# Two-scale attention and two feed-forward layers: first layer in tiles of 288 and 432 tokens, attention pairs in five or six chunks

## The reference

```python
# attention, batch 4, heads 8, seq 576, head_dim 64, all float32
out_d = softmax_attention(mean of 4 tokens of q, k, v)         # 144 x 144 scores per head
out_local = softmax_attention(q, k, v, masked to |i - j| < 4)  # a band around the diagonal
x = repeat(out_d, 4) + out_local                               # -> 2304 tokens x 512
# layer 1: w_in 512 x 2048, w_out 2048 x 512
h = x @ w_in;  x = maximum(0.01 * h, h) @ w_out
# layer 2, weights of the same shapes
h = x @ w_in2; out = (h - tanh(h)) @ w_out2
```

## Time and profile before

| what | us |
|---|---|
| three runs | 952.02, 952.35, 954.28 |
| the profiled execution's own time | 951.99 |
| its span, first to last instruction | 950.2 |
| around the span | 1.8 |
| PE matmul busy | 939.5 |
| layer 1, first to last | 42.98 to 541.24 |

### The profile page before, as it was taken

How to read it: one execution, slowest core, us unless ns; L and a number is a source line. 1 busy time by engine, 2 the same in 40 slices (tenths; PEclk the granted TensorE clock), 3 DMA queues, 4 the chain that set the end, 5 groups by cost and what they waited for, 6 DMA issues and landing times.

```text
span 950.2 us, 19922 instructions
## 1 busy us (share of the span) xinstructions
PE 939.5 (99%) x7026; PEld 883.6 (93%) x7026; DVE 529.2 (56%) x1070; ACT 557.0 (59%) x1351; POOL 403.5 (42%) x343
## 2 busy tenths in 40 slices
PE   8999999999999999999999999999999999999998
PEld 8799999999999999999999989889899898898997
DVE  6744434534543554344236576776666766766764
ACT  5756446445445455463446677665765755755754
POOL 4776428236246164171534567333233233233232
PEclk9999999999999999999999999999999999999999
DMA  7875211210121121102004022000000000000000
GB/s 159 190 200 141 53 27 27 51 44 26 31 51 26 25 51 45 34 1 68 1 2 143 3 67 78 34 1 1 34 0 0 33 0 0 33 0 0 34 1 33
DMA packets 87797, 41.48 MB, mean 44 GB/s; under 512 B 60352, under 2 KB 81344, under 8 KB 87744
## 3 DMA queue, kind: packets, MB, share of 16 engines
q1 hardware_dynamic: 87744, 40.78, 16.3%
HBM read 36.04 MB, written 4.72 MB: 43 GB/s over the span
## 4 chain that ended last, share of the span: by engine, by line
PE 88%; ACT 4%; POOL 3%; DVE 2%; DMA 1%; issue 1%; SPq 0%; ACTq 0%; DVEq 0%; POOLq 0%
PE ph L540 13%; PE ph L542 13%; PE ph L541 13%; PE acc L569 7%; PE acc L571 7%; PE acc L570 7%; PE acc L616 6%; PE acc L617 6%; PE acc L618 6%; PE banks L429 2%; PE banks L466 2%; PE banks L453 1%; PE banks L422 1%; POOL g_lo L1151 1%; POOL w_lo_b L1158 1%
## 5 line engine op out<-in xcount | busy, mean ns | idle before, releaser
L1151 POOL TENSOR_TENSOR g_lo<-scratch,g_hi 128x384 fp32r<-128x384 f32 x96 | 125.8, 1310 | 257.6 <-ACT g_hi L743 257.6
L996 DVE TENSOR_TENSOR ph<-g,ph 128x288 f32<-128x288 f32 x128 | 59.0, 461 | 174.2 <-ACT g L757 173.6
L540 PE MATMUL ph<-x_hi,w_hi_a 128*128 128x288 f32 (+1 forms) x448 | 143.7, 321 | 0.4 <-DVE x_lo L978 0.2
L541 PE MATMUL ph<-x_lo,w_hi_a 128*128 128x288 f32 (+1 forms) x448 | 140.0, 312 | 0.0
L542 PE MATMUL ph<-x_hi,w_lo_a 128*128 128x288 f32 (+1 forms) x448 | 139.9, 312 | 0.0
L1130 POOL TENSOR_TENSOR in_lo<-w_whole,in_hi 128x512 fp32r<-128x512 f32 x64 | 82.7, 1292 | 133.5 <-ACT in_hi L723 133.5
L757 ACT ACTIVATE g<-ph 128x288 f32<-128x288 f32 x128 | 52.5, 410 | 135.2 <-PE ph L542 135.2
L1135 POOL TENSOR_TENSOR out_lo<-w_whole,out_hi 128x512 fp32r<-128x512 f32 x64 | 86.1, 1346 | 71.5 <-ACT out_hi L727 71.4
L1030 DVE SCALAR_TENSOR_TENSOR scratch<-scratch,ph 128x384 f32<-128x384 f32 x96 | 53.2, 554 | 109.7 <-ACT scratch L806 105.1
L805 ACT ACTIVATE scratch<-ph 128x384 f32<-128x384 f32 x96 | 46.8, 487 | 108.6 <-PE ph L542 106.9
L983 DVE TENSOR_TENSOR g_lo<-ph,g_hi 128x288 fp32r<-128x288 f32 x128 | 58.5, 457 | 59.2 <-ACT g_hi L743 59.2
(11 more groups left out here) (277 smaller groups left out, 2649.9 us busy)
## 6 DMA issues: line engine op xcount, KB each, us to landing
out_dram<-o_stage SPq DMA_DIRECT2D x18, 256.0 KB, 2.1
w_whole<-in_moe_w_in_dram SPq DMA_DIRECT2D x16, 256.0 KB, 4.2
w_whole<-in_moe_w_out_dram SPq DMA_DIRECT2D x16, 256.0 KB, 5.2
qn<-in_q_dram SPq DMA_DIRECT2D x26, 144.0 KB
kn<-in_k_dram SPq DMA_DIRECT2D x26, 144.0 KB
v4n<-in_v_dram SPq DMA_DIRECT2D x26, 144.0 KB
vw<-in_v_dram SPq DMA_DIRECT2D x26, 122.5 KB
scratch<-in_moe_w_in_dram SPq DMA_DIRECT2D x8, 256.0 KB, 2.9
```

Of the source, the lines that this page charges most:

```text
L540: pe.matmul(bank, whi, x_hi[:, c, 0:width], start=(c == 0), stop=False)
L541: pe.matmul(bank, whi, x_lo[:, c, 0:width], start=False, stop=False)
L996: dve.tensor_tensor(ph1[:, 1 - f % 2, 0:T1], g1[:, f % 2, :], ph1[:, 1 - f % 2, 0:T1], ALU.max)\
L1151: pool.tensor_tensor(g2_lo[:, f % 3, :], g2[:, f % 2, :], g2_hi[:, f % 3, :].bitcast(F32), ALU.subtract).then_inc(g_lo_done, 1)
```

## The change

- `SIZES` makes layer 1 six tiles, two of 288 columns and four of 432. Every buffer of a tile has 432 columns and is used as far as the tile's width. There are 2304 large matmuls in layer 1 instead of 3072, of the same columns in sum.
- No loops over tiles remain in layer 1 on any engine; SP's loop over pairs is unrolled too. Tile borders go from 7 to 5.
- `later` reads a plan: a pair takes six or five chunks instead of eight groups. 63 chunks fill slots 0 to 62 of the 64 of tiles 0 to 3, so the 288 tiles carry three pairs each instead of two. Each chunk has two halves. On PE the first half stands between `hidden1` and `down1`, the second after `down1`. On ACT the first half stands after `leak`, before `keep_y`, `split_in` and `split_g`; on DVE after the maximum.
- `v4n` and `pT` share memory, and ACT's step 11 waits for POOL's step 5 of the pair.
- No pair begins or ends at a tile's f = 1.

```diff
+SIZES = (288, 288, 432, 432, 432, 432)
+IN_SIX = {
+    "pe": (((0, 1), (2, 3)), ((), (4,)), ((), (6,)), ((), (11, 12)), ((), (13, 14)), ((), (15, 16))),
+    "act": (((0, 1), (2, 3)), NONE, ((7,), (8,)), ((), (11, 12)), ((), (13, 14)), ((), (15,))),
+    "dve": (((), (3,)), ((), (4, 5)), ((8,), (7, 9)), NONE, NONE, ((), (15, 16))),
+    "pool": (NONE, ((), (5,)), ((), (9, 10)), NONE, NONE, NONE),
+}
+IN_FIVE = {
+    "pe": IN_SIX["pe"][:4] + (((13, 14), (15, 16)),),
...
+PLAN = (IN_SIX, IN_FIVE, IN_FIVE) * 2 + (IN_SIX,) + (IN_FIVE,) * 5
...
+        def later(engine, tile, f, half):
+            at = CF * tile + f
+            for pair in range(len(PLAN)):
+                if f < CF and BEGINS[pair] <= at < BEGINS[pair + 1]:
+                    for step in PLAN[pair][engine][at - BEGINS[pair]][half]:
+                        if pair > 0 or step >= HEAD:
+                            yield step, A, pair + 1
...
-            with sp.Fori(1, MIXED) as tile:
-                for par in range(2):
-                    load_qk(A, 2 * tile + 1 + par, 4 * tile + 8 + 2 * par)
-                    load_v(A, 2 * tile + 1 + par, 4 * tile + 8 + 2 * par)
+            for i in range(3, len(PLAN) + 1):
+                load_qk(A, i, 2 * i + 6)
+                load_v(A, i, 2 * i + 6)
...
+            def layer1(tile, ahead):
                 for f in range(CF + LAG1):
-                    if f < CF and not (begun and f == 0):
+                    if 0 < f < CF:
                         hidden1(tile, f)
+                    if f > 0:
+                        for step, s, i in later("pe", tile, f, 0):
+                            attention(step, s, i)
                     if ahead and f == CF + LAG1 - 1:
                         hidden1(tile + 1, 0)
+                        for step, s, i in later("pe", tile + 1, 0, 0):
+                            attention(step, s, i)
                     if f >= LAG1:
                         down1(tile, f - LAG1)
-                    for step, s, i in later(f, tile, last):
+                    for step, s, i in later("pe", tile, f, 1):
                         attention(step, s, i)
...
-            layer1(0, CF)
-            with pe.Fori(1, MIXED - 1) as tile:
-                layer1(tile, CF)
-            layer1(MIXED - 1, CF - GROUP_HEAD)
-            for tile in range(MIXED, TILES1):
-                layer1(tile, 0, ahead=tile < TILES1 - 1)
+            for tile in range(TILES1):
+                layer1(tile, ahead=tile < TILES1 - 1)
...
                 elif step == 11:
+                    act.wait_ge(s.vd_done, i + 1)
                     act.wait_ge(s.bank_full[1], uses1(i, 4))
```

More of the change, by code:

```diff
@@ L85, in two_scale_attention_and_feed_forward, with columns1, pairs_below @@
     WHOLE = CF - KEPT
-    assert D == QB and DM == CD * P and LP * RUN == S and NB * QB == S and PAIRS == 4 + 2 * MIXED
+    assert D == QB and DM == CD * P and LP * RUN == S and NB * QB == S and PAIRS == 4 + len(PLAN)
+    assert sum(SIZES) == TOKENS
+    STARTS = [sum(SIZES[:tile]) for tile in range(TILES1)]
+    BEGINS = [sum(len(plan["pe"]) for plan in PLAN[:pair]) for pair in range(len(PLAN) + 1)]
+    def columns1(tile):
+        return slice(STARTS[tile], STARTS[tile] + SIZES[tile])
+    def pairs_below(tile):
+        return CD * ((STARTS[tile] + SIZES[tile] - 1) // S)
+    for tile in range(1, TILES1):
+        assert BEGINS[pairs_below(tile)] <= CF * tile - 1
     qv = q.rearrange("b h (p r) d -> p (b h) r d", r=RUN)
@@ L184, in two_scale_attention_and_feed_forward, with place_a @@
             w_whole = sb("w_whole", [P, WHOLE, CW], at=first)
-            A = PairBuffers("a", lambda name, shape: sb(name, shape, at=first), banks)
+            v4n_and_pT = sb("v4n_and_pT", [P, NB * P], at=first)
+            def place_a(name, shape):
+                if name in ("v4n", "pT"):
+                    return shaped(v4n_and_pT[0:shape[0], 0:math.prod(shape[1:])], shape)
+                return sb(name, shape, at=first)
+            A = PairBuffers("a", place_a, banks)
             band_r = sb("band", [P, NB, WIN], F32R, at=first)
@@ L553, in hidden1 @@
                 wait_from(pe, g_lo_done, n - 1)
-                hidden(ph1[:, 1 - f % 2, 0:T1], hi, lo, x1_hi, x1_lo, T1, CD * tile if f == 0 else None)
+                width = SIZES[tile]
+                hidden(ph1[:, 1 - f % 2, 0:width], hi, lo, x1_hi, x1_lo, width, CD * tile if f == 0 else None)
             def down1(tile, f):
@@ L742, in split_g @@
                 wait_from(act, y_done, n if f == 0 else n - 2)
[L743 removed]
+                act.activation(g_hi, raw, ACT.Copy).then_inc(g_hi_done, 1)
             def keep_y(tile):
@@ L747, in keep_y, with layer1 @@
                 for c in range(2):
-                    act.activation(xT[:, c, bass.ds(tile * T1, T1)], acc[:, c, 0:T1], ACT.Copy)\
+                    act.activation(xT[:, c, columns1(tile)], acc[:, c, 0:SIZES[tile]], ACT.Copy)\
                         .then_inc(y_kept_act, 1)
-            def layer1(tile, last, extra, keep_before, ahead):
+            def layer1(tile):
+                width, last = SIZES[tile], tile == TILES1 - 1
                 for f in range(CF + 1):
@@ L756, in layer1 @@
                         wait_from(act, g_done, n - 1)
-                        act.activation(g1[:, f % 2, :], ph1[:, 1 - f % 2, 0:T1], ACT.Copy, scale=0.01)\
+                        act.activation(g1[:, f % 2, 0:width], ph1[:, 1 - f % 2, 0:width], ACT.Copy, scale=0.01)\
                             .then_inc(leak_done, 1)
-                    if f == 0:
-                        keep_before()
+                    for step, s, i in later("act", tile, f, 0):
+                        attention(step, s, i)
+                    if f == 0 and tile > 0:
+                        keep_y(tile - 1)
                     if KEPT <= f + 2 < CF:
@@ L763, in layer1 @@
                     if f < CF:
[L764 to L767, removed]
+                        split_g(n, f, ph1[:, 1 - f % 2, 0:width], g1_hi[:, f % 3, 0:width])
+                    if f == CF - 1 and not last:
+                        next_x(tile + 1)
+                    for step, s, i in later("act", tile, f, 1):
                         attention(step, s, i)
-                    extra(f)
-                    if isinstance(tile, int) and tile == 0 and f + 3 < KEPT:
+                    if last:
+                        w2a(f)
+                    if tile == 0 and f + 3 < KEPT:
                         split_kept(f + 3)
@@ L775, in next_x @@
             def next_x(tile):
[L776 to L781, removed]
+                if pairs_below(tile) > 0:
+                    act.wait_ge(A.bank_free[0], uses0(pairs_below(tile) + 1, 0))
+                split_x(x1_hi, SIZES[tile], columns1(tile), CF * tile)
             def nothing(f=None):
@@ L818, in layer2 @@
                     if f:
-                        split_g(N1 + CF * tile + f - 1, f - 1, g2[:, (f - 1) % 2, :], g2_hi)
+                        split_g(N1 + CF * tile + f - 1, f - 1, g2[:, (f - 1) % 2, :], g2_hi[:, (f - 1) % 3, :])
                     extra(f)
-                split_g(N1 + CF * tile + CF - 1, CF - 1, g2[:, (CF - 1) % 2, :], g2_hi)
+                split_g(N1 + CF * tile + CF - 1, CF - 1, g2[:, (CF - 1) % 2, :], g2_hi[:, (CF - 1) % 3, :])
             def keep_out(tile):
@@ L870, in _ @@
             split_kept(EARLY)
[L871 to L879, removed]
+            for tile in range(TILES1):
+                layer1(tile)
+            split_x(x2_hi, T2, slice(0, T2), N1)
             keep_y(TILES1 - 1)
@@ L988, in keep_y, with layer1 @@
                 for c in range(2, CD):
-                    dve.tensor_copy(xT[:, c, bass.ds(tile * T1, T1)], acc[:, c, 0:T1]).then_inc(y_kept_dve, 1)
-            def layer1(tile, last, extra, keep_before, ahead):
+                    dve.tensor_copy(xT[:, c, columns1(tile)], acc[:, c, 0:SIZES[tile]]).then_inc(y_kept_dve, 1)
+            def layer1(tile):
+                width, last = SIZES[tile], tile == TILES1 - 1
                 for f in range(CF + 1):
                     n = CF * tile + f
+                    raw = ph1[:, 1 - f % 2, 0:width]
                     if f < CF:
                         dve.wait_ge(leak_done, n + 1)
[L996 to L999, removed]
+                        dve.tensor_tensor(raw, g1[:, f % 2, 0:width], raw, ALU.max).then_inc(g_done, 1)
+                    for step, s, i in later("dve", tile, f, 0):
+                        attention(step, s, i, (i + 3) // CD, (i + 3) % CD)
+                    if f == 0 and tile > 0:
+                        keep_y(tile - 1)
                     if f < CF:
[L1001 to L1004, removed]
+                        lo_of_g1(n, f, width)
+                    if f == CF - 1 and not last:
+                        lo_of_x(x1_hi, x1_lo, SIZES[tile + 1], columns1(tile + 1), CD * (tile + 1))
+                    for step, s, i in later("dve", tile, f, 1):
```

(19 more changed lines are left out.)

53 lines of the change are left out of this document (28 added, 25 removed).

## The result

The changed kernel takes 943.31 us (median of four runs, 943.01 to 944.20) against 952.62 for the kernel before in the same comparison. The ratio is 0.9902, 95% interval 0.9889 to 0.9914: 9.3 us less. Forecast were 6.2 us less, 946.1, and a range of 942.5 to 951.3. The sign and the range held; the gain is half as large again as the sum.

The account below looks back on a forecast made before the run. PE's matmul stream was taken to bound the kernel; -4.4 (pace) - 1.3 (borders) - 0.5 (end) - 0.8 + 0.8 (attention) = -6.2 us, giving a median of 946.1 us, range 942.5 to 951.3.

Parts of the forecast that it names:

- What bounds the kernel: Whole kernel: PE's stream, busy 99% of the span at 2.4 GHz; other engines' busy time is no cost in itself.
- 1, the pace: Layer 1's large matmuls: 768 fewer and wider ones, 432 columns at an interpolated 196.5 ns; -4.4 us.
- Both bounds: Limits of the pace term: 0 if 432 columns take 199.4 ns, -9.9 us if they take 192.9.
- both rivals about the pace: Excess fixed per matmul: 940.6 us, chance 0.06; pace proportional to columns: 950.5, chance 0.16 together with half-microsecond waits.
- 2, the borders: Tile borders in layer 1: fewer and cheaper; -1.3 us, from 0 to -2.0.
- the longer cover: Borders without attention: the longer hidden product hides more of the chain, so 0.33 us shrinks to about 0.1.
- 3, the end: End of layer 1: the last down product's wait for `out_lo` goes; -0.5 us, from 0 to -0.5.
- 4, attention: Attention pairs in layer 1: a wait for POOL's normalising goes, -0.8 us; new waits in narrow tiles, +0.8.
- their bound of 6 us: Upper bound on attention's new waits: 0.5 us for each of 12 pairs, +6 us.
- The chain: A narrow-tile pair, from scores' end: POOL's normalising done at 6.4 to 6.5 us, PE at step 11 at 7.0.
- the margins of 0.5 us: Slack of attention steps before PE needs them: near 0.5 us or more each, 0.5 at step 11.
- the slower rival: ACT's queue bounds around attention pairs; a microsecond late for all 12 gives +12 us, 958.1; chance 0.08.

Follow-up runs that it names:

- run 5: Changed kernel with seven tiles of 288, 288, 288, 432, 336, 384 and 288 tokens; 947.54 us in one execution.
- run 4: Changed kernel with eight tiles of 288 tokens, every tile buffer laid out for 432 columns; 951.49 us, ratio 0.9974 to the kernel before.
- run 6: Changed kernel with two tiles of 288 tokens and eight of 216; 996.89 us in one execution.
- run 1: Kernel before with every loop over layer 1's tiles unrolled on all engines, nothing else; 954.13 us, ratio 1.0008 to the kernel before.
- run 2: Changed kernel with eight tiles of 288 tokens: new plan, no loops, old width; 951.86 us, ratio 0.9986 to the kernel before.
- run 7: Changed kernel with the transposes of q and k in one block behind the down product, on PE and ACT; 951.52 us, ratio 0.9982 to the kernel before.
- run 8: Changed kernel with the plan shifted by one slot so that one pair begins at f = 1 of the second tile; 944.64 us in one execution.
- run 10: Changed kernel with POOL's two normalising steps (9 and 10) one chunk later; 973.06 us, ratio 1.0198 to the kernel before.
- run 9: Changed kernel with eight tiles of 288 tokens, v4n and pT in separate memory, ACT's wait for `vd_done` gone; 953.07 us in one execution.

## Why the prediction was right, and where its sum was off

- **What bounds the kernel:** right. PE's stream, at one clock, before and after.
- **1, the pace:** the mechanism right, the size too small. "432 should take 175.8 + 48 x 0.432 = 196.5 ns" failed: 195.4. It was interpolated between two rows of layer 2, where 384 columns take 1.0 to 1.3 ns more than in layer 1 (run 5); with layer 1's 174.5 in place of 175.8 the same interpolation gives 195.7. With 195.4 the term is 3072 x 132.9 - 768 x 132.9 - 1536 x 195.4 = -6.1 instead of -4.4. The narrow tiles' 0.3 ns (run 4) adds 0.2. Both bounds and both rivals about the pace are excluded: a cycle per column would be 192.9, proportion 199.4. The line through 132.8 ns at 288 columns and 195.4 at 432 leaves 7.6 ns at zero columns. That is where the line points and not a part of a matmul that a run shows by itself; the line holds only above some width, and 216 columns stand 10 ns over it (run 6). The Trainium skill ("TensorE: Matmul & The Clock Gate", section "Back-to-back issue gap") gives N / 2.4 + 2.5 ns for a warm matmul. The trace doesn't agree: 288 columns stand 12.8 ns over N / 2.4 and 432 stand 15.4, and the 1.9 us that this would have made of the term is out.
- **2, the borders:** right for those without attention. The two hidden products before the first down product of tile 4 take 388.33 - 383.54 = 4.79 us, 4.69 by the pace: 0.1 over, as forecast for the longer cover:

```profile
383.54 0.37 PE L576 MATMUL ph<-x_hi,w_hi_a 128*128 128x432 f32 x1
...
388.33 0.36 PE L608 MATMUL acc<-g_hi,w_hi_a 128*128 128x432 f32 x1
```

  For those with attention 0.18 each was too much: the first such border (112.81 to 118.24, less the 0.47 of an attention block and two switches of 0.1) is within 0.1 of the pace. So are the other two by the same working (184.91 to 191.11, 279.93 to 287.61). That makes some 0.5 us. A tile in a loop takes 0.16 us longer than unrolled (run 1). The Trainium skill ("Runtime: NRT & Kernel Launch", section "Instruction fetch mechanics") says that a taken branch out of the fetched window stalls the fetch; the sign agrees, but no run parts the fetch from whatever else a loop costs.
- **3, the end:** right, and a little more. The last three down products (524.43 to 531.47) take 7.04 us, 36 x 195.4 is 7.03; the wait of the earlier trace rows is gone. Before they took 5.55 (535.69 to 541.24) for 4.78 by the pace, so what went was 0.8 and not 0.5.
- **4, attention:** the wait that goes did go (run 2). "So I take 0.2 us for each of the four five-chunk pairs" and their bound of 6 us failed: no wait of PE is left in layer 1 that wasn't there before. The chain was worked out to within 0.1 us up to POOL's end, and PE came 0.2 later than forecast, so the margin was 0.8; the margins of 0.5 us did hold, and a further 0.8 us on top of them was caution without a row. Runs 7, 8 and 10 show that the slower rival's mechanism exists and what it costs where a step stands in the wrong place; the plan avoids it.
- **Not foreseen:** layer 2 took 0.8 us more in this profile. From its first hidden product to its last matmul it took 405.4 to 407.0 us in all twelve profiles, without any relation to the change, and the difference lies in its first tile, which loads and splits weights. Waits for POOL's `g_lo` there are 0.4 of it. I count it as scatter.

In sum layer 1 gained 10.0 us where 6.2 were forecast. Of the 3.8 between, 1.7 and 0.2 are pace, 0.8 waits that didn't come, 0.5 borders and 0.3 the end; 0.3 are left, of which the first pair's shorter wait for POOL (0.25 for 0.45) is 0.2. All of these lie on one side, so no error of the sum hid another. Layer 2's scatter takes 0.8 back in this profile, and by that much the result is nearer to the forecast by chance.

## What to carry to other kernels

Where PE is the bound, take the time from start to start by width, in the same stage of the kernel, draw the line through two widths, and multiply what it leaves at zero columns by the count of matmuls that go; here 7.6 ns by 768, 5.8 of the 6.1 us. It holds between measured widths only: 216 columns took near 112 ns. A wider tile needs its inputs earlier, and the plan that makes that possible can cost more than the width brings: keep a wide matmul group between two dependent attention blocks, and put the step that another engine waits for ahead of that engine's routine work, not behind it. Write down every instruction in the queue ahead of a moved step, those of the slot before too.

## What the runs showed of the hardware that was not expected

- The layout of SBUF buffers alone changes the pace of matmuls: 51.37 against 51.49 us for 384 matmuls of 288 columns, in each tile alike (run 4). Only the hidden products gain, 133.1 to 132.5 ns; which buffer does it was not tried.
- PE's granted clock can be halved for 3.4 or 6.8 us after a wait of a few microseconds, and the work behind the wait then costs as much again. In run 10 it fell at the end of or right after waits of 5.46, 3.48, 3.48 and one of 2.25 us (PE back at 62.56, 93.90, 174.90 and 201.90), and not at another of 2.25 (back at 122.10); in batch 0 it fell after one of 1.98 (run 9) and not after one of 1.48 (run 1). The rows give no length of wait that decides.
- Matmuls of 216 columns start 111.7 ns apart, as if of some 240 columns by the line; 288, 336, 384 and 432 lie on one line (132.8, 154.0, 174.5, 195.4).
- Hidden products of 384 columns take 175.5 ns a matmul in layer 2 and 174.5 in layer 1, in one execution (run 5). Why was not tried.
